# The second tile's rows, softmax and convolution moved earlier in the head of a fused convolution and two feed-forward layers

## The chip, the cores and the metric

The kernel runs on one core of a Trainium2 chip. The metric is the device time of one execution in microseconds, the median of some runs without a profile. The profile comes from one further execution.

## The reference

`x` is (2, 4096, 192), `weight_gen` is (2, 4096, 8, 7). Each token gets eight heads of seven weights, which a softmax normalises; the output of the first stage is a causal convolution over seven tokens with these weights. Two feed-forward layers follow, all in float32:

```
w = exp(weight_gen - max); w = w / (sum(w) + 1e-9)              # over the 7 taps
out[b,s,h,:] = sum_k w[b,s,h,k] * x_pad[b,s+k,h,:]              # 8 heads of 24 columns
h = max(out @ w_in, 0);  x1 = (h*h) @ w_out                     # 192 -> 2048 -> 192
h = x1 @ w_in2;          y  = (h*cos(h)) @ w_out2               # 192 -> 2048 -> 192
```

## The kernel before

The 8192 tokens are cut into 16 tiles of 512 (`TILES`, `TOK`). A tile is convolved and transposed, so that the 192 columns lie on partitions, and goes through the first layer in 16 chunks of 128 hidden columns (`SLOTS`); the second layer's chunks of the same tile run 19 slots behind (`LAG`). A slot `n` holds the up-projection of chunk `n` of layer 1, a down-projection of an earlier chunk of layer 1 and, from slot 19 on, the same for layer 2. To get float32 accuracy each operand is split into a high and a low half (`_hi`, `_lo`), and three products of halves are summed. TensorE does most matmuls on half of its rows, 64 each (`half`, L608).

Each engine has its own queue, in an order written out by hand in the loops over slots; semaphores tie them. In the first 19 slots (the head) there is no second layer, and the other engines have one-off work between the slots:

- **VectorE** starts with the softmax of `weight_gen` parts 0 and 1 (tiles 0 and 1), convolves tile 0 (`convolve_first`, L1426 and L1433), subtracts the first weight pieces' low halves (L1545, L1549) and makes the two low halves of x1 of tile 0 (L1553). Then per slot: the square of the relu (L1458, except for `ACT_SQUARES`, which ScalarE squares) and the low half of the chunk (`low`, L1507), and behind each slot what `CONV_AFTER` lists (the convolution of tile 1, `convolve_second`: products at L1401, sums at L1410, the running sum being in the PSUM tensor y1) and what `SOFTMAX_AFTER` lists (`softmax(part, op)`: op 0 the maximum, 1 the subtraction, 2 the sum, 3 add 1e-9 and take the reciprocal, 4 the scaling, L1387).
- **ScalarE** makes the relu, the high halves and the exponentials, and rounds the weight pieces (`piece_his`, L1126).
- **GpSimd** makes the low halves of the weight pieces (`piece_lo`: L562, L564, L566, L568 for each of 16 pieces), subtracts maxima (`shift`) and convolves the tiles from 2 on.
- **SP** issues most DMAs in one order: gen part group 0, rows of x of tile 0, weight pieces 0 to 3, gen group 1, the rows of tile 1 (`load_rows(1)`), pieces 4 and 5, gen group 2, further pieces. `load_rows(1)` waits until all seven products of `convolve_first` have read the same buffer `xc`, `load_rows(2)` for tile 1's last sum (`x1_ready`). `load_piece(pc)` waits until GpSimd is done with piece `pc - 4`.
- **TensorE** runs three chunks alone (`up_alone`: slots 0 to 2), then `head_slot`, which waits at its start for low n-3 of the chunk whose down-projection it holds (`downs_of_slot`: `g1_ready`). At the end of slot `turn_at(0)` it transposes tile 1 (`turn_x1`, L725, 16 instructions), for which it waits for `x1_ready`. `split_at(0)`, slot 13, is where ScalarE and VectorE split the transposed tile.

The first chunk uses x1's halves as they come (L635 to L652). Its waits on `x1_split` are for the two subtractions of VectorE at L1553; the matmul shown is L644:

```
pe.wait_ge(x1_hi_ready, 1)
...
pe.wait_ge(x1_split, 1)
pe.matmul(o, wa_hi[l][:, f_cols], xa_lo[l][:, par, :], start=False, stop=False)
...
pe.wait_ge(x1_split, 2)
```

Of the kernel before, what the change touches and what calls it, by code (L numbers as in the profile page):

```python
# [7 lines left out]
def conv_ffn_ffn_kernel(nc, x_d, gen_d, w_in1_d, w_out1_d, w_in2_d, w_out2_d, out_dram):  # L8
# [18 lines left out]
    SLOTS = FF // P  # L27
# [13 lines left out]
    TURN = 3  # L41
# [20 lines left out]
    PEEL = 2  # L62
# [20 lines left out]

    def turn_at(t):

        return (SLOTS - 3, SLOTS - 9)[t] if t < PEEL else TURN

    def split_at(t):

# [22 lines left out]
    with ctx:  # L112
# [137 lines left out]
        LATE = 4  # L250

        ACT_SQUARES = (2, 3, 4, 5, 6, 7, 8)
        CONV_SLOTS = (1, 1, 2, 2, 3, 4, 5, 6, 7, 8, 9, 10, 11)

# [7 lines left out]
        for k in range(TAPS):  # L264
            for op in range(2 if k else 1):
                CONV_AFTER.setdefault(CONV_SLOTS[2 * k - 1 + op if k else 0], []).append((k, op))

# [1 line left out]

        PARTS = [0] + [JJ * t for t in range(1, TILES + 1) if t == 1 or t % 2 == 0]  # L270
        LOADS = [0, 2, 5, len(PARTS) - 1]
        SOFTMAX_AFTER = {0: [(1, 2), (1, 3), (1, 4)]}
        SOFTMAX_AFTER.update({n: [(n - 1, 0)] for n in range(3, 10)})
        SOFTMAX_AFTER.update({12: [(2, 2)], 13: [(2, 3)]})
        SOFTMAX_IN = {29: [(3, 2)], 30: [(3, 3)]}
        SOFTMAX_IN.update({2 * SLOTS + (6, 7, 9, 10, 11, 12, 13, 14, 15, SLOTS + 6)[k]: [(4 + k // 2, 2 + k % 2)]
# [51 lines left out]
        def stat_view(part):  # L328
            a, b = gen_range(part)
            return stat[:, a * HEADS:b * HEADS]  # L330
# [44 lines left out]
        def load_first_own(eng, quarters):  # L375

            for q in quarters:
                eng.dma_start(xc[q * BLOCK:(q + 1) * BLOCK, HALO * DM:],  # L378
                              x_v[:, q * JJ * DM:(q + 1) * JJ * DM]).then_inc(x_own, 16)
# [31 lines left out]
        def store_a(eng, t, r, blocks):  # L411
            eng.wait_ge(out_a_ready, t + 1)
            tokens = slice(t * QUARTERS * JJ, (t + 1) * QUARTERS * JJ)
            for d in blocks:
                cols = slice(d * BLOCK, (d + 1) * BLOCK)
                eng.dma_start(out_v[:, tokens, cols],
                              out_a[r][cols, :].rearrange("n (j c) -> n j c", c=BLOCK)).then_inc(stored[r], 16)

        def store_d(eng, t, r, blocks):
            eng.wait_ge(out_d_ready, t + 1)  # L420
            half = QUARTERS * JJ // 2
            for k in blocks:
                j0 = t * QUARTERS * JJ + k * BLOCK // DD * half
                col = DA + k * BLOCK % DD
                eng.dma_start(out_v[:, j0:j0 + half, col:col + BLOCK],
                              out_d[r][k * BLOCK:(k + 1) * BLOCK, :].rearrange("n (j c) -> n j c", c=BLOCK)
                              ).then_inc(stored[r], 16)

        def load_gen(eng, r, quarters=range(QUARTERS)):
            part_a, part_b = LOADS[r], LOADS[r + 1]  # L430
            t0, t1 = PARTS[part_a] // JJ, PARTS[part_b] // JJ
            for q in quarters:
                eng.dma_start(gen[q * BLOCK:(q + 1) * BLOCK, PARTS[part_a] * GEN:PARTS[part_b] * GEN].rearrange(  # L433
                                  "p (t k) -> p t k", t=t1 - t0),
                              gen_v[:, t0:t1, q, :]).then_inc(gen_loaded[r], 16)

        @block.sync
        def _(sp):
            def load_piece(pc):
                l, q = divmod(pc, PL)  # L440
                r = pc % RING
                if pc >= RING:
                    sp.wait_ge(piece_ready[pc - RING], 3)
                cols = slice(q * PIECE, (q + 1) * PIECE)
                sp.dma_start(stage_a[:, r, :], w_in_d[l][0:DA, cols]).then_inc(piece_loaded[r], 16)
                sp.dma_start(stage_d[l * DD:(l + 1) * DD, r, :], w_in_d[l][DA:DM, cols]).then_inc(piece_loaded[r], 16)
                sp.dma_start(stage_o[:, r, :, :],
                             w_out_v[l][:, q * PF:(q + 1) * PF, :]).then_inc(piece_loaded[r], 16)

            def load_rows(c):  # L450
                if c == 1:
                    sp.wait_ge(first_product, TAPS)
                else:
                    sp.wait_ge(x1_ready, c - 1)
                sp.wait_ge(x_loaded, FIRST_X + NEXT_X * (c - 1))
                for q in range(QUARTERS):
                    at = ((c * QUARTERS + q) * JJ - HALO) * DM
                    sp.dma_start(xc[q * BLOCK:(q + 1) * BLOCK, :], x_v[:, at:at + ROWS * DM]).then_inc(x_loaded, 16)

            def move_blocks(t):  # L460

                sp.wait_ge(blocks_ready, t - 1)
                blocks = x_blocks[:, :].rearrange("p (j d n) -> p j d n", j=JJ, n=BLOCK)
                for d in range(DM // BLOCK):
                    for q in range(QUARTERS):
                        cols = slice(q * P, (q + 1) * P)
                        to = xt_a[d * BLOCK:(d + 1) * BLOCK, cols] if d < DA // BLOCK else \
                            xt_d[d * BLOCK - DA:(d + 1) * BLOCK - DA, cols]
                        sp.dma_start(to.rearrange("p (j n) -> p j n", j=JJ),
                                     blocks[q * BLOCK:(q + 1) * BLOCK, :, d, :]).then_inc(blocks_moved, 16)  # L470

            load_gen(sp, 0, (0, 1))
            load_first_own(sp, (0, 1))
            load_first_halo(sp, ((1, B), (0, 0), (0, 1), (1, 0), (1, 1)))
            for pc in range(RING):
                load_piece(pc)
            load_gen(sp, 1)
            load_rows(1)
            for pc in range(RING, RING + 2):
                load_piece(pc)  # L480
            load_gen(sp, 2)
            for pc in range(RING + 2, PL + 4):
                load_piece(pc)
            load_rows(2)
            for pc in range(PL + 4, PIECES):
                load_piece(pc)
            load_rows(3)
            move_blocks(2)
            for t in range(2, TILES + 2):
                if t + 2 < TILES:  # L490
                    load_rows(t + 2)
                if t + 1 < TILES:
                    move_blocks(t + 1)

                blocks = range(4 if t <= TILES else 2)
                store_a(sp, t - 2, t % 2, blocks)
                store_d(sp, t - 2, t % 2, blocks)
            for r in range(2):
                sp.wait_ge(stored[r], STORE * (TILES // 2))
# [802 lines left out]
        def _(dve):  # L1302
            def softmax(part, op):

                if op == 0:
                    dve.wait_ge(gen_loaded[sum(part >= a for a in LOADS[1:])], 16 * QUARTERS)
                    dve.tensor_reduce(stat_view(part), gen_view(part), axis=AX.X,
                                      op=ALU.max).then_inc(gen_max[part], 1)
                elif op == 1:
                    dve.wait_ge(gen_max[part], 1)  # L1310
                    dve.tensor_tensor(gen_view(part), gen_view(part), spread(part),
                                      ALU.subtract).then_inc(gen_shifted, 1)
                elif op == 2:
                    dve.wait_ge(gen_exp, part + 1)
                    dve.tensor_reduce(stat_view(part), gen_view(part), axis=AX.X,
                                      op=ALU.add).then_inc(gen_sum[part], 1)
                elif op == 4:
                    scale(part)
                else:
                    dve.wait_ge(gen_sum[part], 1)  # L1320
                    dve.tensor_scalar(stat_view(part), stat_view(part), 1e-9, None,
                                      ALU.add).then_inc(gen_sum[part], 1)
                    dve.wait_ge(gen_sum[part], 2)
                    dve.reciprocal(stat_view(part), stat_view(part)).then_inc(inv_ready, 1)
# [214 lines left out]
            for op in range(2, 4):  # L1539
# [8 lines left out]
            dve.wait_ge(piece_ready[0], 1)  # L1548
            dve.tensor_tensor(wd_lo[0:DD, 0:PIECE], stage_d[0:DD, 0, :], wd_hi[0:DD, 0:PIECE],  # L1549
                              ALU.subtract).then_inc(piece_ready[0], 1)  # L1550
            for part in range(2):
                dve.wait_ge(x1_hi_ready, part + 1)
                dve.tensor_tensor(by_half(x1_low(0, part)), x1_source(0, part), by_half(x1_high(0, part)),  # L1553
                                  ALU.subtract).then_inc(x1_split, 1)
            for n in range(TAIL):
# [4 lines left out]
                for k, op in CONV_AFTER.get(n, ()):  # L1560
                    convolve_second(k, op)
                for part, op in SOFTMAX_AFTER.get(n, ()):
                    softmax(part, op)
# [31 lines left out]
```

## Time and profile before

| | us |
|---|---|
| median of 3 runs | 1176.63 (1176.55 to 1176.8) |
| the profiled execution's own time | 1176.54 |
| its span, first to last instruction | 1174.7 |
| TensorE busy | 1167.3 (99%) |
| VectorE busy | 961.2 (82%) |
| ScalarE busy | 805.9 (69%) |
| GpSimd busy | 367.1 (31%) |

A span is the time from the first to the last instruction of the core; the execution's own time also has what lies around it. Shares are of the span. Engines overlap, so their busy times do not add up; the end of a matmul is modelled. The granted TensorE clock is 0.999 of full speed over the span.

### The profile page before, as it was taken

What the parts mean: (1) busy time and instruction counts of PE and PEld (TensorE: products, weight loads), DVE (VectorE), ACT (ScalarE), POOL (GpSimd) and SP (SyncE); (2) the same over time, 40 slices, a digit from 0 to 9 for tenths busy, and PEclk for the clock granted to TensorE, in tenths of its full rate; (3) what the DMA queues carried; (4) which work ended last, traced back from release to release, by engine and by line L of the source; (5) the groups of instructions that cost most, each with busy time, mean ns of one, the idle gap of its engine ahead of it and who ended that gap; (6) DMA issues with size and microseconds to landing.
All of it is one profiled execution on the core that took longest, in us unless ns stands there. A gap on an engine that the chain in (4) does not pass through costs nothing.

```text
span 1174.7 us, 25693 instructions
## 1 busy us (share of the span) xinstructions
PE 1167.3 (99%) x9906; PEld 1129.7 (96%) x9906; DVE 961.2 (82%) x1505; ACT 805.9 (69%) x1467; POOL 367.1 (31%) x265
## 2 busy tenths in 40 slices
PE   9999999999999999999999999999999999999998
PEld 7989999999999999999999999999999999999987
DVE  7968898878778787887878878787787878878787
ACT  5977766666666676666766666676666766666676
POOL 4994634070420606025070430705215070000000
PEclk9999999999999999999999999999999999999999
DMA  8511111110111101111011111101111000100001
GB/s 212 138 48 31 37 27 35 25 35 10 23 35 29 35 11 18 35 28 35 15 24 29 25 35 28 35 9 21 35 29 35 13 17 3 26 2 15 1 1 28
DMA packets 113173, 37.32 MB, mean 32 GB/s; under 512 B 101662, under 2 KB 110878, under 8 KB 113052
## 3 DMA queue, kind: packets, MB, share of 16 engines
q1 hardware_dynamic: 111100, 34.87, 14.3%
q8 instruction: 79, 1.29, 0.5%
q10 hardware_dynamic: 1952, 0.80, 0.3%
q14 instruction: 42, 0.34, 0.1%
HBM read 23.84 MB, written 6.29 MB: 26 GB/s over the span
## 4 chain that ended last, share of the span: by engine, by line
PE 99%; DVE 0%; ACT 0%; ACTq 0%; issue 0%
PE y L608 51%; PE h L608 46%; PE y L713 1%; PE h L637 0%; ACT L1131 0%; PE h L630 0%; PE y L674 0%; DVE tap L1426 0%; PE h L644 0%; PE h L640 0%; ACTq L378 0%; ACTq L389 0%; ACTq L433 0%; PE y L676 0%; PE y L675 0%
## 5 line engine op out<-in xcount | busy, mean ns | idle before, releaser
L608 PE MATMUL y<-g_hi,wo 64*128 64x512 f32 x3048 | 695.1, 393 | 0.2
L608 PE MATMUL y<-g_lo,wo 64*128 64x512 f32 x2032 | 515.9, 391 | 0.0
L608 PEld LDWEIGHTS y<-g_hi,wo 64*128 64x128 f32 x3048 | 414.3, 184 | 14.1 <-PE y L608 1.1
L529 POOL TENSOR_TENSOR tap<-xc,gen 128x768 f32<-128x768 f32 x98 | 151.3, 1550 | 575.4 <-DVE xd_lo L1513 555.3
L608 PEld LDWEIGHTS y<-g_lo,wo 64*128 64x128 f32 x2032 | 298.6, 184 | 1.7
L1167 ACT ACTIVATE turns<-turns 128x512 f32<-128x512 f32 x238 | 150.2, 631 | 182.6 <-DVE turns L1464 182.6
L608 PE MATMUL h<-xa_hi,wa_hi 64*128 64x512 f32 x1018 | 267.6, 397 | 0.1
L608 PE MATMUL h<-xa_hi,wa_lo 64*128 64x512 f32 x1018 | 262.7, 391 | 0.0
L608 PE MATMUL h<-xa_lo,wa_hi 64*128 64x512 f32 x1018 | 262.3, 391 | 0.0
L1484 DVE TENSOR_TENSOR h<-h,turns 128x512 f32<-128x512 f32 x238 | 165.6, 696 | 114.7 <-ACT turns L1167 114.2
L1458 DVE SCALAR_TENSOR_TENSOR h<-h,relu 128x512 f32<-128x512 f32 x249 | 173.4, 696 | 56.5 <-ACT relu L1142 54.3
L1180 ACT ACTIVATE g_hi<-h 128x512 fp32r<-128x512 f32 x238 | 142.6, 599 | 87.7 <-DVE h L1484 87.7
L1142 ACT ACTIVATE relu<-h 128x512 f32<-128x512 f32 x256 | 152.5, 596 | 62.8 <-PE h L608 62.2
L1494 DVE SCALAR_TENSOR_TENSOR g_lo<-h,g_hi 128x512 fp32r<-128x512 f32 x238 | 164.6, 692 | 18.8 <-ACT g_hi L1180 0.9
L1507 DVE TENSOR_TENSOR g_lo<-h,g_hi 128x512 fp32r<-128x512 f32 x256 | 174.3, 681 | 2.2 <-ACT g_hi L1192 1.2
L1464 DVE SCALAR_TENSOR_TENSOR turns<-h,turns 128x512 f32<-128x512 f32 x238 | 162.3, 682 | 1.4 <-ACT turns L1152 1.0
L1192 ACT ACTIVATE g_hi<-relu 128x512 fp32r<-128x512 f32 x256 | 158.0, 617 | 0.4
L608 PEld LDWEIGHTS h<-xa_lo,wa_hi 64*128 64x128 f32 x1018 | 149.1, 184 | 0.5
L608 PEld LDWEIGHTS h<-xa_hi,wa_lo 64*128 64x128 f32 x1018 | 149.2, 184 | 0.4
L1152 ACT ACTIVATE turns<-h 128x512 int32<-128x512 f32 x238 | 141.9, 596 | 1.2 <-PE h L608 1.2
L608 PEld LDWEIGHTS h<-xa_hi,wa_hi 64*128 64x128 f32 x1018 | 129.1, 184 | 12.3 <-issue 2.1
L608 PE MATMUL h<-xd_hi,wd_hi 64*128 64x512 f32 x513 | 133.3, 392 | 0.0
(124 smaller groups left out, 1076.0 us busy)
## 6 DMA issues: line engine op xcount, KB each, us to landing
xc<-in_x_dram SPq DMA_DIRECT2D x60, 240.0 KB
out_dram<-arena SPq DMA_DIRECT2D x62, 64.0 KB, 1.9
xt_a<-x_blocks SPq DMA_DIRECT2D x224, 16.0 KB, 1.8
arena<-in_moe_w_out_dram SPq DMA_DIRECT2D x16, 192.0 KB, 3.3
arena<-in_moe_w_in_dram SPq DMA_DIRECT2D x16, 128.0 KB, 2.6
out_dram<-arena SPq DMA_DIRECT2D x62, 32.0 KB, 1.7
xt_d<-x_blocks SPq DMA_DIRECT2D x112, 16.0 KB, 1.8
arena<-in_moe_w_in_dram SPq DMA_DIRECT2D x16, 64.0 KB, 2.9
```

What stands on the lines that cost most here:

```text
L529: pool.tensor_tensor(tap[:, k % 2, :].rearrange("p (r g) -> p r g", g=GROUP), rows[k], wk, ALU.mult).then_inc(pool_step, 1)
L608: return pe.matmul(o, w[rows, :], x[rows, :], start=start, stop=stop)
L1142: act.activation(relu[:, b, :], h1_bank(n), ACT.Relu).then_inc(relu_done, 1)
L1152: act.activation(turns[:, c, :], h2[c], ACT.Copy, bias=0.25).then_inc(turns_ready, 1)
L1167: act.activation(wave[:, c, :], wave[:, c, :], ACT.Sin, scale=2.0 * math.pi).then_inc(cos_ready, 1)
L1180: act.activation(g2_hi[:, c, :], h2[c], ACT.Copy, scale=2.0 * math.pi).then_inc(g2_hi_ready, 1)
L1192: act.activation(g1_buffers(n)[0], relu[:, n % 2, :], ACT.Square).then_inc(g1_hi_ready, 1)
L1458: dve.scalar_tensor_tensor(h1_bank(n), h1_bank(n), 0.0, relu[:, b, :], ALU.max, ALU.mult).then_inc(square_ready, 1)
L1464: dve.scalar_tensor_tensor(wave[:, c, :], h2[c], 0.25, turns[:, c, :], ALU.add, ALU.subtract).then_inc(fraction_ready, 1)
L1484: dve.tensor_tensor(h2[c], h2[c], wave[:, c, :], ALU.mult).then_inc(g2_made, 1)
L1494: dve.scalar_tensor_tensor(g2_lo[:, c, :], h2[c], 2.0 * math.pi, g2_hi[:, c, :], ALU.mult, ALU.subtract).then_inc(g2_ready, 1)
L1507: dve.tensor_tensor(lo, h1_bank(n), hi, ALU.subtract).then_inc(g1_ready, 1)
```

## The change

SP issues the rows of tile 1 ahead of gen group 1. VectorE does the last three softmax operations of part 1 (four instructions) before the low halves of tile 0's x1 instead of behind slot 0. The convolution of tile 1 begins behind slot 0 with three operations, has two behind slot 1 and one behind each of slots 2 to 9 (before: two behind slot 1, two behind slot 2, one behind each of slots 3 to 11). TensorE's transposes of tile 1 come behind slot 12 instead of 13.

```diff
     def turn_at(t):
 
-        return (SLOTS - 3, SLOTS - 9)[t] if t < PEEL else TURN
+        return (SLOTS - 4, SLOTS - 9)[t] if t < PEEL else TURN
...
-        CONV_SLOTS = (1, 1, 2, 2, 3, 4, 5, 6, 7, 8, 9, 10, 11)
+        CONV_SLOTS = (0, 0, 0, 1, 1, 2, 3, 4, 5, 6, 7, 8, 9)
...
-        SOFTMAX_AFTER = {0: [(1, 2), (1, 3), (1, 4)]}
-        SOFTMAX_AFTER.update({n: [(n - 1, 0)] for n in range(3, 10)})
+        SOFTMAX_AFTER = {n: [(n - 1, 0)] for n in range(3, 10)}
...
             for pc in range(RING):
                 load_piece(pc)
+            load_rows(1)
             load_gen(sp, 1)
-            load_rows(1)
...
             dve.tensor_tensor(wd_lo[0:DD, 0:PIECE], stage_d[0:DD, 0, :], wd_hi[0:DD, 0:PIECE],
                               ALU.subtract).then_inc(piece_ready[0], 1)
+            for op in range(2, 5):
+                softmax(1, op)
             for part in range(2):
                 dve.wait_ge(x1_hi_ready, part + 1)
```

## Rows read from the trace of the kernel before

**Rows 1.** The page, busy us, share of the span, instructions
```profile
PE 1167.3 (99%) x9906; PEld 1129.7 (96%) x9906; DVE 961.2 (82%) x1505; ACT 805.9 (69%) x1467; POOL 367.1 (31%) x265
```

**Rows 2.** Busy time by stretch: us from:to, length, busy of each engine, clock
```profile
22.00:62.00 40.00, 40.00 (x304) 36.02 (x304) 36.71 (x52) 35.88 (x74) 37.28 (x47) 1.00 0.66 158
62.00:75.00 13.00, 12.65 (x80) 9.04 (x79) 8.33 (x12) 10.22 (x18) 12.53 (x8) 1.00 0.10 28
75.00:1110.00 1035.00, 1035.00 (x8865) 1015.91 (x8867) 848.56 (x1326) 705.49 (x1276) 310.39 (x197) 1.00 0.12 24
```

**Rows 3.** Timeline of VectorE, 13 to 24 us: start, duration, line, operands, idle before
```profile
13.55 0.95 DVE L1426 TENSOR_TENSOR tap<-xc,gen 128x768 f32<-128x768 f32 x1
...
16.00 0.42 DVE L1549 TENSOR_TENSOR wd_lo<-arena,wd_hi 64x256 fp32r<-64x256 f32 x1
17.13 0.69 DVE L1553 TENSOR_TENSOR xa_lo<-y,xa_hi 128x512 fp32r<-128x512 f32 x1 [0.71 <-ACT xa_hi L1273]
...
20.71 0.69 DVE L1507 TENSOR_TENSOR g_lo<-h,g_hi 128x512 fp32r<-128x512 f32 x1
21.32 0.38 DVE L1315 TENSOR_REDUCE stat<-gen 128x32 f32<-128x224 f32 x1
...
22.38 0.39 DVE L1387 TENSOR_TENSOR gen<-gen,stat 128x224 f32<-128x224 f32 x1
22.69 0.69 DVE L1458 SCALAR_TENSOR_TENSOR h<-h,relu 128x512 f32<-128x512 f32 x1
23.42 0.69 DVE L1507 TENSOR_TENSOR g_lo<-h,g_hi 128x512 fp32r<-128x512 f32 x1
```

**Rows 4.** Line L1321 over the whole span: duration in ns, least, median, most
```profile
L1321 DVE TENSOR_SCALAR stat<-stat x9: 181/223/1573, 5.7 to 226.6; 128x64 f32<-128x64 f32 x7, 128x32 f32<-128x32 f32 x2
```

**Rows 5.** Timeline of TensorE: the first chunk's matmul of xa_lo
```profile
18.02 0.40 PE L644 MATMUL h<-xa_lo,wa_hi 128*128 128x512 f32 x1
```

**Rows 6.** Timeline of GpSimd, 16 to 26 us
```profile
16.50 0.72 POOL L562 TENSOR_TENSOR wa_lo<-arena,wa_hi 128x256 fp32r<-128x256 f32 x1 [13.93 <-DVE wd_lo L1549]
17.37 0.74 POOL L564 TENSOR_TENSOR wd_lo<-arena,wd_hi 64x256 fp32r<-64x256 f32 x1
18.08 0.45 POOL L566 TENSOR_TENSOR wo<-arena,wo 128x128 fp32r<-128x128 f32 x1
18.49 0.74 POOL L568 TENSOR_TENSOR wo<-arena,wo 128x256 fp32r<-128x256 f32 x1
...
22.06 0.46 POOL L566 TENSOR_TENSOR wo<-arena,wo 128x128 fp32r<-128x128 f32 x1
...
24.22 1.35 POOL L564 TENSOR_TENSOR wd_lo<-arena,wd_hi 64x256 fp32r<-64x256 f32 x1
```

**Rows 7.** Timeline of VectorE, 24 to 31 us
```profile
24.89 1.50 DVE L1401 TENSOR_TENSOR tap<-xc,gen 128x768 f32<-128x768 f32 x1
...
29.56 0.68 DVE L1507 TENSOR_TENSOR g_lo<-h,g_hi 128x512 fp32r<-128x512 f32 x1
30.16 0.95 DVE L1410 TENSOR_TENSOR y<-y,tap 128x768 f32<-128x768 f32 x1
```

**Rows 8.** Timeline of TensorE: first up-projection matmul of slots 4, 5 and 6
```profile
25.28 0.39 PE L608 MATMUL h<-xa_hi,wa_hi 64*128 64x512 f32 x1
...
27.85 0.39 PE L608 MATMUL h<-xa_hi,wa_hi 64*128 64x512 f32 x1
...
30.49 0.47 PE L608 MATMUL h<-xa_hi,wa_hi 64*128 64x512 f32 x1
```

**Rows 9.** Timeline of SP's queue: the gen loads and the rows of tile 1
```profile
12.25 3.23 SPq L433 DMA_DIRECT2D gen<-in_weight_gen_dram  x4
15.60 1.76 SPq L458 DMA_DIRECT2D xc<-in_x_dram  x4
```

**Rows 10.** Timeline: VectorE's last sum of tile 1, TensorE's transposes
```profile
49.74 0.95 DVE L1410 TENSOR_TENSOR x<-y,tap 128x768 f32<-128x768 f32 x1
...
50.96 0.67 PE L725 MATMUL y<-ident,x 64*128 64x64 f32 x14
```

## The prediction

> **What bounds the kernel now.** I read the page's busy shares first: TensorE is busy 1167.3 of 1174.7 us [rows 1]. Busy time by stretch comes next: from 22 to 62 us and from 75 to 1110 us it has no gap, 40.00 of 40.00 and 1035.00 of 1035.00 us [rows 2]. The order written out by hand is the same from 75 us on, so the change can act only on the head. There TensorE is a fixed chain of matmuls, and whatever delays one of them for lack of input stays in the end time: behind 22 us there is nothing idle to absorb it but 0.35 us between 62 and 75 us [rows 2], which is the second layer's starting chain. So the question is whether VectorE, which gives TensorE the low halves, is later or earlier than before for chunks 0 to 3. Times here are of the profiled execution: 1176.54 us, span 1174.7; the median of the plain runs is 1176.63, 0.09 more.
>
> I call "low n" the subtraction at L1507 that ends chunk n's low half. TensorE's slot n+3 needs low n.
>
> **How VectorE and GpSimd meet.** A product of 128x768 takes 0.95 us while GpSimd is idle (13.55 [rows 3]); the second product of tile 1 took 1.50 us, 24.89 to 26.39 [rows 7]. GpSimd's L564 takes 0.74 us alone and took 1.35, 24.22 to 25.57 [rows 6]. These fit one reading: only one of them runs at a time. L564 started while the first product ran and waited for it; the second product then waited for L564 until 25.44, which is 0.13 before L564's reported end, and ran its 0.95 to 26.39. Subtractions and additions with an operand in PSUM do not wait (low 3 at 29.56, 0.68; the addition at 30.16, 0.95, GpSimd being busy beside both [rows 7]). The small TENSOR_SCALAR at L1321 took 181 ns at best and 1573 at worst [rows 4], so it waits too, with one operand only.
>
> The Trainium skill, "SBUF — State Buffer", section "SBUF: two separate sides", calls the port pair that VectorE and GpSimd share "an exclusive lock, not a bandwidth split", taken by a VectorE operation with two SBUF inputs or in a two-port mode. The rows above agree. Without such a lock the sum below would be 0.9 us; with it, it is 2.9. That the lock speaks against this change is my main reason.
>
> **Softmax ahead of the low halves of x1 (adds four operations, takes them from slot 0).** VectorE sits between wd_lo (16.00) and xa_lo (17.13) with 0.71 us idle [rows 3], waiting for ScalarE. The four operations took, start to start, 21.32 to 22.69 = 1.37 us (the last, 22.38, overlaps the next by 0.08) [rows 3]. Without GpSimd: they start at 16.34 (wd_lo's 0.42 less 0.08 overlap), so xa_lo starts at 17.71, 0.58 late. With the lock: GpSimd's L562 runs 16.50 to 17.22 and L564 17.37 to 18.11 [rows 6]. The TENSOR_SCALAR, due at 16.76, waits until 17.09 and ends at 17.27; the reciprocal runs 17.31 to 17.66; the scaling multiply, due at 17.70, waits for L564 until 17.98 and ends at 18.37. xa_lo then starts at 18.29, 1.16 late. TensorE's L644 started at 18.02, 0.20 behind xa_lo's end at 17.82 [rows 3, 5], and all that follows is in its queue. **Term 1: +1.16 us (bounds 0.58 and 1.16).** What the cover was worth: 0.71 of the softmax is hidden, the rest is paid by the first chunk. Chunk 1 gains from it, since the softmax stood between its low 0 and low 1, but nothing waited there.
>
> **Three convolution operations in slot 0, two in slot 1.** Before, low 0 (20.71) was followed by the softmax, square 1 and low 1 (23.42 to 24.11) [rows 3]; slot 4 began at 25.28 [rows 8]. From low 3 (ends 30.24) to the matmul at 30.49 [rows 7, 8] the handover takes 0.25 us; slots are 2.57 apart when nothing waits (25.28 to 27.85) and slot 6 was 2.64 behind slot 5 [rows 8], followed by a restart that costs 0.08 more. So slot 4 had 25.28 - 24.36 = 0.92 in hand.
> Now walk it, GpSimd's list shifted by 0.14 (the scaling multiply holds L566 back from 18.08 to 18.22 [rows 6]):
> - Low 0 starts at 20.71 + 1.16 = 21.87, the first product is due 0.61 later, 22.48. L566 (22.06 + 0.14 = 22.20) holds the port until 22.53. Product 22.53 to 23.48.
> - GpSimd's L568, 0.74 us, came at 22.61 and waited to 23.33; it lets go at 23.94. Second product to 24.89.
> - The addition of two SBUF buffers needs both (24.93); L562 has gone ahead at 24.74 until 25.34. Addition to 26.29.
> - Square 1 from 26.21, low 1 0.73 later, 26.94 to 27.63. Slot 4 can begin at 27.88; without the wait it would at 25.28 + 1.16 = 26.44. **Term 2: +1.44, and 0.08 for the restart.** Lower bound, three operations unstretched (0.86, 0.99, 0.86 start to start): with term 1 at 0.58, low 1 ends at 26.03, slot 4 waits 0.42 + 0.08.
> - Slot 1: the product is due at 27.55, waits for L566 and L568 (27.43) until 28.04, ends 28.99; the addition into PSUM 29.03 to 29.98; low 2 29.89 to 30.58. Slot 5 at 30.83 against 27.88 + 0.08 + 2.57 = 30.53. **Term 3: +0.30 and 0.08** (bounds: nothing, 0.4).
> - Slot 2 has one operation where it had two: low 3 starts at 31.36, ends 32.05; slot 6 is due at 30.83 + 2.65 = 33.48, so it does not wait. **Term 4: -0.16**, the stall and restart of slot 6 before.
> From slot 3 the operations are one per slot as before, two slots ahead, and low 4 has over a microsecond in hand.
> Sum: 1.16 + 1.52 + 0.38 - 0.16 = **+2.9 us**.
>
> **Rows of x ahead of weight_gen.** SP issued the four gen loads in 12.25 to 15.48 and the rows in 15.60 to 17.36 [rows 9]. Now SP stands at the wait for the seventh product, which ends at 13.55 + 0.95 = 14.50 [rows 3]: 2.25 us in which nothing is issued, behind it the gen loads, piece 4 and all later pieces. Rows go out at 14.6 to 16.4, gen to 19.6, piece 4 from 19.7. The landing of rows has no row of its own. Before, the first product (right behind low 1's 0.61 us, so 24.03) found them landed, at most 6.7 us behind the last issue at 17.36; now that bound gives 23.0 against the need at 22.48: cost 0 to 0.5, and I take 0, since the queue ahead is shorter. gen is first read behind slot 3, about 32 us: nothing. Piece 4 comes a few tenths later; ScalarE, which converts it, is not what low 3 waits for now. Cost 0, at most 0.3.
>
> **Transposes behind slot 12 instead of 13.** Tile 1's last sum ended at 49.74 + 0.95 = 50.69, and the 16 transposes began at 50.96 [rows 10], where TensorE had just run out of the slot's matmuls: 0.02 of handover room, no stall. The same 16 instructions are paid one slot earlier. The sum now ends two slots earlier, some 47 us, ahead of their place at about 51. 0 us (bounds -0.3, +0.1). Chunk 13's result comes half a microsecond later to ScalarE, which runs behind there anyway. The second tile's rows (load_rows(2), behind this sum) go out earlier, which nothing waited for.
>
> **Rivals.**
> 1. *The first product gets the port first.* If term 1 is 0.65 (the scaling multiply slips in ahead of L564), the product is due at 21.97, before L566. The same walk gives product to 22.92, second to 24.05, addition to 25.46, low 1 to 26.80, slot 4 at 27.05 against 25.93: 1.12 + 0.08; slot 5 is not late. 0.65 + 1.20 - 0.16 = +1.7: 1178.3 us. For it: two instructions 0.3 us apart decide. Against it: L564 had a start 0.33 ahead.
> 2. *No stretching at all*: 0.58 + 0.50 - 0.16 = +0.9: 1177.5. Against it the 1.50 and 1.35 us rows.
> 3. *Larger*: the rows are late by 0.5, or one more operation is held by GpSimd (0.5): +3.4: 1180.0.
> 4. *Other side*: the extra 0.5 us around the transposes was partly a wait for the sum. Slots 13 and 14 would have to give back more than the head costs; the price is at most 0.3 there and 0.16 at slot 6, and it decides only if the head costs less than 0.46, that is if the softmax hides wholly in the 0.71 idle: 1176.2. Against it 1.37 > 0.71.
>
> **Numbers.** Forecast 1176.6 + 2.9 = 1179.5 us, chance 0.52; rival 1 0.24, rival 2 0.12, rival 3 0.09, rival 4 0.03. What a measurement here can tell from no change is about 0.2%, 2.35 us. The forecast's own range, 1179.1 to 1180.0, lies above 1178.98 nearly whole; slower by over that 0.58, within it 0.41, faster 0.01. Range 1177.6 to 1180.2.
>
> **What would show it.** xa_lo at 18.3 instead of 17.13, L644 at 19.2; L1321 and L1387 longer than 0.2 and 0.39. The first product at 22.5, low 1 ending near 27.6, TensorE waiting 1.4 us before slot 4 for L1507. Slot 6 some 3.0 later than 30.49, and the same shift at the end. Wrong if the products beside GpSimd keep 0.95, if slot 4 does not wait, or if the shift at slot 6 is given back later.

## The result: slower by 8 us, by an operation that took nine times its length, and by the clock

| | median us | runs, us |
|---|---|---|
| before | 1176.62 | 1176.37 to 1177.24 (6) |
| changed | 1184.58 | 1181.36 to 1186.49 (6) |
| ratio | 1.0064 | 95% interval 1.0053 to 1.0075 |

The forecast was 1179.5 (range 1177.6 to 1180.2). The sign came out as forecast, the size did not, and the runs now spread over 5 us where they had spread over 1. Line numbers after 272 are one lower in the changed kernel (L1386 is L1387 before).

The page's busy shares look like those of [rows 1]:

```profile
PE 1170.9 (99%) x9906; PEld 1130.2 (96%) x9906; DVE 963.6 (82%) x1505; ACT 806.2 (68%) x1467; POOL 366.6 (31%) x265
```

TensorE is busy 3.6 us more with the same matmuls, the first hint. VectorE ahead of the first chunk, in the changed kernel's timeline (start, duration, line, operands, idle before):

```profile
16.17 0.42 DVE L1548 TENSOR_TENSOR wd_lo<-arena,wd_hi 64x256 fp32r<-64x256 f32 x1
16.51 0.37 DVE L1314 TENSOR_REDUCE stat<-gen 128x32 f32<-128x224 f32 x1
16.92 0.51 DVE L1320 TENSOR_SCALAR stat<-stat 128x32 f32<-128x32 f32 x1
17.47 0.35 DVE L1323 RECIPROCAL stat<-stat 128x32 f32<-128x32 f32 x1
17.86 1.17 DVE L1386 TENSOR_TENSOR gen<-gen,stat 128x224 f32<-128x224 f32 x1
19.06 0.69 DVE L1554 TENSOR_TENSOR xa_lo<-y,xa_hi 128x512 fp32r<-128x512 f32 x1
```

GpSimd at the same time:

```profile
17.54 0.73 POOL L563 TENSOR_TENSOR wd_lo<-arena,wd_hi 64x256 fp32r<-64x256 f32 x1
18.24 0.45 POOL L565 TENSOR_TENSOR wo<-arena,wo 128x128 fp32r<-128x128 f32 x1
18.65 0.96 POOL L567 TENSOR_TENSOR wo<-arena,wo 128x256 fp32r<-128x256 f32 x1
```

The scaling multiply, 0.39 us long in [rows 3], took 1.17: it stood from 17.86 until 18.64 (19.03 less 0.39) and was passed by L565. So xa_lo began at 19.06, against 17.13 [rows 3]. TensorE:

```profile
19.80 0.50 PE L643 MATMUL h<-xa_lo,wa_hi 128*128 128x512 f32 x1 [1.39 <-DVE xa_lo L1554]
...
21.13 0.79 PE L636 MATMUL h<-xa_hi,wa_hi 128*128 128x512 f32 x1
...
24.28 0.79 PE L636 MATMUL h<-xa_hi,wa_hi 128*128 128x512 f32 x1
...
30.14 0.39 PE L607 MATMUL h<-xa_hi,wa_hi 64*128 64x512 f32 x1
...
35.27 0.39 PE L607 MATMUL h<-xa_hi,wa_hi 64*128 64x512 f32 x1
```

The first row answers to [rows 5]: 19.80 against 18.02, 1.78 late, behind a gap of 1.39 us. The last two answer to [rows 8]: slot 4 is 4.86 late, slot 6 4.78, and the span is 4.7 longer (1179.4 against 1174.7). Between the first chunk and slot 4 another 3.08 us went, but not by waiting: the matmuls grew to 0.79 us. Busy time and granted clock by stretch (from:to, length, busy of PE, PEld, DVE, ACT, POOL, then the clock) show why:

```profile
19.00:20.00 1.00, 0.20 (x1) 0.19 (x1) 0.97 (x3) 0.37 (x1) 1.00 (x3) 1.00 0.85 169
20.00:21.00 1.00, 1.00 (x4) 0.48 (x3) 0.34 (x1) 0.00 (x0) 1.00 (x3) 1.00 1.06 217
21.00:22.00 1.00, 1.00 (x3) 0.78 (x3) 0.14 (x1) 0.73 (x2) 0.86 (x2) 0.54 1.14 223
...
27.00:28.00 1.00, 1.00 (x8) 0.80 (x6) 0.96 (x3) 0.46 (x1) 1.00 (x2) 0.55 1.13 215
28.00:29.00 1.00, 1.00 (x8) 0.77 (x6) 1.00 (x2) 0.97 (x3) 0.20 (x1) 1.00 1.12 237
```

From 21.1 to 27.9 us (0.54 and 0.55 being mixtures) the granted clock is 0.50, that is 1.2 GHz instead of 2.4. TensorE counts as wholly busy there; only the clock column gives it away. A share of busy time would have hidden it.

This profile is of the fastest of the six executions. What the others lost is the first question to the experiments.

### The profile page after: what moved, and what is told of

It is laid out like the page before. It is cut to its first block, busy times and chain, and to the rows that moved or that the text cites. A ratio compares the mean times of both kernels' runs of the same rounds, so it can differ in the third digit from the quotient of the medians.

```text
span 1179.4 us, 25693 instructions
## 1 busy us (share of the span) xinstructions
PE 1170.9 (99%) x9906; PEld 1130.2 (96%) x9906; DVE 963.6 (82%) x1505; ACT 806.2 (68%) x1467; POOL 366.6 (31%) x265
## 4 chain that ended last, share of the span: by engine, by line
PE 98%; DVE 1%; DMA 0%; SPq 0%; issue 0%; ACT 0%; DVEq 0%
PE y L607 51%; PE h L607 46%; DMA xc<-in_x_dram 0%; DVE tap L1425 0%; PE h L636 0%; PE h L643 0%; SPq L391 0%; DVE gen L1386 0%; PE h L639 0%; DVE tap L1432 0%; PE y L673 0%; DVE turns L1432 0%; DVE relu L1425 0%; DVE turns L1425 0%; SPq L377 0%
```

## The experiments

Theory A: the softmax ahead of xa_lo makes TensorE wait, and the gap lets the clock fall. Theory B: the early convolution makes the loss. After the first four runs theory A got a third part, called C: VectorE gets the shared port only in a pause of GpSimd's work. A filler is a matmul whose result nobody reads (L629, `keep_busy`).

| kernel | median us (range, runs) | ratio to before, 95% |
|---|---|---|
| softmax ahead, nothing else changed | 1185.62 (1184.38 to 1187.35, 4) | 1.0075 (1.006 to 1.009) |
| changed, softmax behind the low halves | 1181.40 (1181.25 to 1182.71, 5) | 1.0038 (1.0023 to 1.0052) |
| changed, 6 fillers | 1184.70 (1183.32 to 1186.26, 4) | 1.0066 (1.0051 to 1.0081) |
| changed, GpSimd starts behind the multiply | 1178.39 (1178.24 to 1179.06, 10) | 1.0013 (1.0004 to 1.0023) |
| changed, a gap in GpSimd's work | 1179.39 (1179.08 to 1182.32, 7) | 1.0027 (1.0015 to 1.0038) |
| softmax ahead, GpSimd starts behind the multiply | 1178.01 (1177.59 to 1178.32, 10) | 1.0008 (0.9998 to 1.0017) |
| changed, 17 fillers | 1181.37 (1181.32 to 1181.64, 5) | 1.0036 (1.0023 to 1.0049) |
| rows of x first, nothing else | 1176.71 (1176.40 to 1177.54, 10) | 1.0000 (0.999 to 1.0009) |
| changed, twice more | 1184.57, 1187.24 | |
| early convolution without the softmax's move | 1182.15 (1181.42 to 1183.12, 4) | 1.0044 (1.0029 to 1.0059) |
| transposes earlier, nothing else | 1178.18 (1177.79 to 1181.32, 10) | 1.0015 (1.0005 to 1.0024) |

The kernel before ran beside them at 1176.85, 1176.87 and 1176.98 us.

**1. Only the softmax moved.**

```diff
-        SOFTMAX_AFTER = {0: [(1, 2), (1, 3), (1, 4)]}
...
+            for op in range(2, 5):
+                softmax(1, op)
             for part in range(2):
                 dve.wait_ge(x1_hi_ready, part + 1)
```

> The kernel before with one part of the change: the three softmax operations of part 1 stand ahead of the low halves of x1; rows, convolution and transposes are where they were. Theory A (the head's wait and the clock): TensorE waits for xa_lo 1.3 to 1.8 us longer than before, and the granted clock then falls to half for about 6 us, which costs another 3 us or more: 1181 to 1185 us, all or nearly all of the change's loss. Theory B (the early convolution and its wait ahead of slot 4 make the loss, and the clock fell because of the sum of waits): here at most the wait for xa_lo, +1.8 us, 1178.4 us, clock 0.999.

1185.62 us: theory A (0.6 us above its range). The move of four small operations alone loses as much as the whole change. Its timeline has the multiply and what TensorE then waited, and the stretch from 23 to 36 us the clock, 0.50 throughout:

```profile
17.61 3.54 DVE L1386 TENSOR_TENSOR gen<-gen,stat 128x224 f32<-128x224 f32 x1
...
21.93 0.51 PE L643 MATMUL h<-xa_lo,wa_hi 128*128 128x512 f32 x1 [3.77 <-DVE xa_lo L1554]
```

```profile
23.00:36.00 13.00, 13.00 (x42) 8.64 (x42) 7.71 (x9) 6.34 (x12) 6.03 (x9) 0.50 0.77 173
```

I had expected at most 1.8 us of waiting here; it was 3.8. The multiply can wait much longer than in the first profile.

**2. The changed kernel twice more.** No edit.

> The changed kernel, unaltered, for one more profile. Theory C says that its first profile (1181.4 us, the multiply at L1386 taking 1.17 us) was one of the short waits and that most executions have the long one: near 1184.5 us, the multiply 3.5 us, TensorE's gap near 3.7 us, the granted clock at half for over 10 us. If the other executions lost their time elsewhere, the multiply is again near 1.2 us and the gap near 1.4.

> The same once more, with the same expectations: the multiply near 3.5 us and 1184.5 us in most executions, near 1.2 us and 1181.4 us in a few.

Both had the long wait. From the first of them, VectorE's multiply, GpSimd beside it, and TensorE:

```profile
17.81 3.53 DVE L1386 TENSOR_TENSOR gen<-gen,stat 128x224 f32<-128x224 f32 x1
18.20 0.44 POOL L565 TENSOR_TENSOR wo<-arena,wo 128x128 fp32r<-128x128 f32 x1
18.61 0.71 POOL L567 TENSOR_TENSOR wo<-arena,wo 128x256 fp32r<-128x256 f32 x1
19.29 0.45 POOL L565 TENSOR_TENSOR wo<-arena,wo 128x128 fp32r<-128x128 f32 x1
19.70 0.71 POOL L567 TENSOR_TENSOR wo<-arena,wo 128x256 fp32r<-128x256 f32 x1
20.38 0.71 POOL L561 TENSOR_TENSOR wa_lo<-arena,wa_hi 128x256 fp32r<-128x256 f32 x1
21.24 0.72 POOL L563 TENSOR_TENSOR wd_lo<-arena,wd_hi 64x256 fp32r<-64x256 f32 x1
22.12 0.80 PE L643 MATMUL h<-xa_lo,wa_hi 128*128 128x512 f32 x1 [3.81 <-DVE xa_lo L1554]
```

The multiply ended at 21.34, so it was let in at 20.95: just when L561 (20.38 to 21.09) was done. Behind L561 there is a pause of 0.15 us, since L563 waits for L561's own semaphore. The five instructions from 18.20 to 20.38 follow each other without any, and all of them passed the waiting multiply. The two executions differ in the clock: half from 20.6 to 30.8 us in the first (1184.57), from 20.0 to 37.1 in the second (1187.24), worked out from the shares of single microseconds. The first stands at the median of the six runs, 1184.58, so of the typical loss 4.1 us is waiting (22.12 against 18.02), and the other 3.9 us arises behind it, where the clock is at half.

**3. A gap in GpSimd's work.** The same instructions in the same order; GpSimd only waits for its own L563 before L565.

```diff
                 piece_lo(1, op)
+            pool.wait_ge(piece_ready[1], 2)
             piece_lo(0, 2)
```

> The changed kernel with one more wait on GpSimd: behind L563 of piece 1 it waits for that instruction's own semaphore before L565 of piece 0, which leaves the sequence of instructions as it is but opens a gap of some 0.15 us between the two. Theory C (VectorE gets the shared port only in a gap between GpSimd's instructions, and GpSimd's back-to-back instructions keep it): the multiply at L1386 is let in at that gap, takes 0.4 to 0.8 us instead of 1.2 to 3.6, xa_lo starts near 18.3, TensorE's gap is about 0.7 us, and the time is 1178.0 to 1180.0 us. If arbitration is by chance or by order of arrival, the multiply varies as before and the median stays at 1182 to 1186 us.

```profile
17.29 0.74 POOL L563 TENSOR_TENSOR wd_lo<-arena,wd_hi 64x256 fp32r<-64x256 f32 x1
18.10 0.49 POOL L565 TENSOR_TENSOR wo<-arena,wo 128x128 fp32r<-128x128 f32 x1
...
17.60 0.67 DVE L1387 TENSOR_TENSOR gen<-gen,stat 128x224 f32<-128x224 f32 x1
...
19.05 0.50 PE L644 MATMUL h<-xa_lo,wa_hi 128*128 128x512 f32 x1 [0.85 <-DVE xa_lo L1555]
27.82 0.47 PE L608 MATMUL h<-xa_hi,wa_hi 64*128 64x512 f32 x1 [1.24 <-DVE g_lo L1507]
33.25 0.39 PE L608 MATMUL h<-xa_hi,wa_hi 64*128 64x512 f32 x1
```

As theory C said: the multiply takes 0.67, and 5.2 us of the median are back (1184.58 to 1179.39), by one semaphore wait that adds no work. The multiply and L565 both wait for L563 here, and the multiply goes first. In this profile L644 is 1.03 late, slot 4 2.54, slot 6 2.76. Three of the seven runs had a mean clock of 0.995 to 0.997 and took 1180.5 to 1182.3: the clock still fell now and then.

So a pause is enough at this place. As a rule theory C does not hold: elsewhere a waiting VectorE operation was let in where GpSimd makes no pause. In the kernel before:

```profile
26.67 0.73 POOL L568 TENSOR_TENSOR wo<-arena,wo 128x256 fp32r<-128x256 f32 x1
26.91 1.32 DVE L1410 TENSOR_TENSOR y<-tap 128x768 f32<-128x768 f32 x1
27.37 1.45 POOL L562 TENSOR_TENSOR wa_lo<-arena,wa_hi 128x256 fp32r<-128x256 f32 x1
```

In the kernel with only the rows of x first (experiment 7), where it is the same multiply behind slot 0:

```profile
22.50 0.74 POOL L568 TENSOR_TENSOR wo<-arena,wo 128x256 fp32r<-128x256 f32 x1
22.59 0.90 DVE L1387 TENSOR_TENSOR gen<-gen,stat 128x224 f32<-128x224 f32 x1
23.19 0.89 POOL L562 TENSOR_TENSOR wa_lo<-arena,wa_hi 128x256 fp32r<-128x256 f32 x1
```

In both, GpSimd's next instruction was issued without a pause and was the one held (1.45 and 0.89 us instead of 0.73). Of some hundred such waits of VectorE between 14 and 80 us in the fourteen profiles, all but seven ended at GpSimd's first change of instruction, a third of them without a pause. The seven are the softmax operations beside GpSimd's first row of instructions, from 17.6 to 21.2 us. What sets that row apart was not tested.

**4. GpSimd starts behind the multiply**, in the changed kernel and in experiment 1's.

```diff
             pool.wait_ge(piece_ready[0], 2)
+            pool.wait_ge(gen_scaled, 2)
```

> The changed kernel with GpSimd's first piece work waiting until the softmax's scaling multiply has ended. Theory A, with the shared port as the cause of the long softmax: the multiply at L1386 takes 0.39 us instead of 1.17 and the TENSOR_SCALAR at L1320 0.18 instead of 0.51; xa_lo starts near 17.9 instead of 19.06, TensorE's gap is 0.4 to 0.6 us instead of 1.39. If so short a gap leaves the clock alone, 1177.5 to 1179 us; if it falls all the same, 1180 to 1184 us. If GpSimd is not the cause, the multiply still takes over 1 us.

> The kernel before with the softmax operations ahead of the low halves of x1 and GpSimd's first piece work waiting for the scaling multiply; rows, convolution and transposes as before. Theory C with the early convolution as a second, separate cost: L644 starts 0.4 us later than before and slot 4 does not wait, 1176.9 to 1177.4 us; the difference to the changed kernel with the same wait on GpSimd (1178.4) is the price of the early convolution, 1.0 to 1.5 us. If the convolution's place costs nothing, it is 1178.4 here too.

In the changed kernel:

```profile
16.62 0.18 DVE L1321 TENSOR_SCALAR stat<-stat 128x32 f32<-128x32 f32 x1
...
17.23 0.39 DVE L1387 TENSOR_TENSOR gen<-gen,stat 128x224 f32<-128x224 f32 x1
...
18.39 0.49 PE L644 MATMUL h<-xa_lo,wa_hi 128*128 128x512 f32 x1 [0.21 <-DVE xa_lo L1555]
27.24 0.47 PE L608 MATMUL h<-xa_hi,wa_hi 64*128 64x512 f32 x1 [1.31 <-DVE g_lo L1507]
```

With GpSimd idle both operations have their short durations, L644 is 0.37 late, and all ten runs keep the clock (0.999 or 1.0). What is left of the loss, 1.6 us, arises at slot 4: 27.24 is 1.96 late.

The second kernel was to give the early convolution's price by difference. It does not: at 1178.01 it is only 0.4 us better, and above what I expected. L644 was 0.58 late in its profile. Slot 6 was 0.63 late there, so slot 4 did not wait, as expected; but the second layer's first chunk was 1.76 late (70.64 against 68.88), again behind a VectorE operation held by GpSimd, further on:

```profile
68.55 2.04 DVE L1531 TENSOR_TENSOR xd_lo<-y_part,xd_hi 64x512 fp32r<-64x512 f32 x1
...
70.64 0.50 PE L637 MATMUL h<-xa_hi,wa_hi 128*128 128x512 f32 x1 [0.68 <-DVE xd_lo L1531]
```

L1531 has two SBUF operands and took 2.04 us instead of 0.69, beside one 1.54 us instruction of GpSimd's convolution of tile 2, which had started 0.05 us earlier. The 1.6 us at slot 4 are read from the slot, not from the two medians.

**5. Fillers, to take away TensorE's gap but not its wait.**

```diff
                 if first:
-                    keep_busy(1)
+                    keep_busy(17)
                     pe.wait_ge(x1_split, 1)
```

> The changed kernel with six filler matmuls instead of one in front of the first chunk's wait for xa_lo (five more of 0.23 us, some 1.2 us, in what was a 1.4 us gap). Theory A, with the gap in TensorE's work as the cause of the clock's fall: the clock stays at 1.0 through 17 to 30 us though xa_lo comes as late; lost are 1.8 us of waiting and 0.3 to 1.4 us ahead of slot 4: 1178.7 to 1179.8 us. If the clock falls for another reason, it falls here too and the time is 1181 to 1185 us.

> The changed kernel with 17 filler matmuls instead of one ahead of the wait for xa_lo, 3.7 us more of them. Theory C: the multiply at L1386 takes as long as before (up to 3.6 us), so the first chunk is still some 3.8 us late, but TensorE has nearly no gap; if the gap is what lets the granted clock fall, it stays at 1.0 and the time is 1180.0 to 1181.8 us. If the clock falls all the same, 1184 to 1187 us.

With 6 (`keep_busy(6)` at the same place) the time was in the range expected if the clock falls for another reason, but the run cannot tell: the multiply took 3.55 us in its profile, a gap of 2.56 us was left, and the clock fell behind it. With 17:

```profile
17.59 3.61 DVE L1386 TENSOR_TENSOR gen<-gen,stat 128x224 f32<-128x224 f32 x1
...
21.97 0.50 PE L643 MATMUL h<-xa_lo,wa_hi 128*128 128x512 f32 x1 [0.18 <-DVE xa_lo L1554]
30.25 0.47 PE L607 MATMUL h<-xa_hi,wa_hi 64*128 64x512 f32 x1 [0.74 <-DVE g_lo L1506]
```

and the same stretch table for 17 to 30 us:

```profile
17.00:30.00 13.00, 12.14 (x56) 8.23 (x54) 11.27 (x13) 7.57 (x17) 8.99 (x15) 1.00 1.09 236
```

xa_lo is 3.95 late as in experiment 2, the clock is 1.00 all through, and all five runs lie within 0.4 us. 1184.58 to 1181.37: on balance the clock costs 3.2 us of the typical loss, and the scatter was its too. Slot 4 now waits 1.0 us more (30.25 - 25.28 - 3.95), which the slow clock had covered; in the main this is why 3.2 is less than the 3.9 of experiment 2.

**6. Softmax between the low halves and slot 0.** The changed kernel with the two lines below the loop instead of above it.

```diff
-            for op in range(2, 5):
-                softmax(1, op)
             for part in range(2):
...
+            for op in range(2, 5):
+                softmax(1, op)
```

> The changed kernel, but with the three softmax operations behind the low halves of x1 and ahead of slot 0. Theory A: TensorE's first chunk is as before (L644's matmul near 18.0 us), the clock stays at 1.0, and what is left is VectorE's first slots: 0 to 0.3 us from the softmax running into square 0, and 0.4 to 1.4 us in front of slot 4: 1176.9 to 1178.3 us. Theory B: no better than the changed kernel, 1181 to 1185 us.

The first chunk was as before, but the 1.5 us of idle VectorE did not hold the softmax: now the TENSOR_SCALAR stood behind four of GpSimd's instructions in a row, square 0 and low 0 came late, and slot 4 waited 2.48 us, in which the clock fell to 0.50:

```profile
18.81 2.33 DVE L1320 TENSOR_SCALAR stat<-stat 128x32 f32<-128x32 f32 x1
...
28.92 0.76 PE L607 MATMUL h<-xa_hi,wa_hi 64*128 64x512 f32 x1 [2.48 <-DVE g_lo L1506]
```

Theory A's range (to 1178.3) was missed by 3 us, by the same error as in experiment 1: I had the operation wait for one instruction at most.

**7. The other parts alone.**

```diff
+                if n == 0:
+                    for op in range(2, 5):
+                        softmax(1, op)
                 for k, op in CONV_AFTER.get(n, ()):
```

is the changed kernel with the softmax back behind slot 0;

```diff
+            load_rows(1)
             load_gen(sp, 1)
-            load_rows(1)
```

is the kernel before with the rows first, and the last one is the kernel before with `turn_at(0)` at slot 12.

> The changed kernel with the softmax operations back behind slot 0, ahead of the convolution's first three operations there: rows, convolution and transposes as changed, the first chunk as before. The head's wait is gone; low 1 is late by the softmax (1.4 us) and three operations (2.7 to 3.7 us), so TensorE waits 2.3 to 3.6 us in front of slot 4. If the clock stays: 1178.8 to 1180.4 us; if a gap this long lets it fall, as the gap ahead of the first chunk did, 1182 to 1184 us. If the early convolution costs nothing: 1176.9 us.

> The kernel before with only the DMA order changed: rows of tile 1 ahead of gen group 1. All theories: nothing waits for either, 1176.4 to 1177.2 us, no difference that can be told. If the rows' place mattered (a later piece 4 holding up ScalarE and slot 6), 1177.5 us or more.

> The kernel before with the transposes of tile 1 behind slot 12 instead of 13, all else as it was. The convolution still ends two operations later than slot 9, behind slot 11, at about 50.7 us, which is 2.3 us after slot 12's place at 48.4: TensorE waits for it, 1178.6 to 1179.2 us. This tells that the transposes could not have been moved without the convolution. If TensorE does not wait, 1176.9 us.

The first matmul of slot 4 in the first, and of the transposes in the last:

```profile
28.74 0.47 PE L607 MATMUL h<-xa_hi,wa_hi 64*128 64x512 f32 x1 [3.16 <-DVE g_lo L1506]
```

```profile
50.94 0.37 PE L725 MATMUL y<-ident,x 64*128 64x64 f32 x2 [2.29 <-issue]
```

The early convolution costs by itself when the softmax stands behind slot 0: slot 4 waits 3.16 us and the clock falls (0.50 at 30 to 31 us), 1182.15 us. The rows' order costs nothing. The transposes could only move because the convolution had; alone they wait 2.29 us, and in some of the ten runs the clock falls behind that too (1177.8 with it at 1.0, up to 1181.3 at 0.998). The median, 1178.18, is below the expected 1178.6 to 1179.2: in the runs at full clock less than half of the 2.29 us shows in the time, and where the rest is regained stays open.

## Why the prediction was wrong

- **What bounds the kernel** was right: all of the loss arises ahead of 38 us, and slot 6's shift (4.78 in the profile) is the end's (4.7). Nothing was given back.
- **The shared port** was read rightly as exclusive, and as holding the one-operand TENSOR_SCALAR (0.51 forecast 0.51: due at 16.92, let in when L561 ended).
- **Term 1 is the step that failed**: "the scaling multiply, due at 17.70, waits for L564 until 17.98". It took for granted that the waiting operation is next when the running instruction ends. Instead GpSimd's L565, L567, L565, L567 and L561 followed without a pause and went first: 3.5 us in five of six profiles with the multiply ahead of xa_lo and GpSimd's sequence untouched, 1.17 in the other. Term 1 measured 1.8 to 4.3 us for 1.16. With a pause of 0.15 us at that place (experiment 3) the multiply took 0.67 and L644 was 1.03 late, and the rest of the sum followed: slot 4 2.54 late (2.60 plus 0.08 forecast), the end 2.6 (2.9), 1179.4 us (1179.5). In the kernel before, each wait of this kind ended at GpSimd's first change of instruction, without a pause too (26.91 above), so the rule was taken from true cases; none of them stood beside GpSimd's first row of instructions. Why the rule fails there stays open.
- **The clock has no term in the prediction**, which is its second error, 3.2 us at the median. I priced a gap as its own length. The kernel before has no gap of over 0.4 us between 17 us and its last matmul, so no row there showed what one does. Experiment 5 shows it: the same wait for xa_lo with the gap filled keeps the clock.
- **Terms 2 and 3**, the wait ahead of slot 4 (1.44 and 0.08) and 5: in the changed kernel's own profile slot 4 does not wait (4.86 of its 4.86 us are older), because TensorE at half speed no longer outruns VectorE. Where the clock stayed, the wait was there: 1.5 us in experiment 3, 1.6 in 4, 1.0 in 5. Slot 5's 0.38 was 0.2 in experiment 3. So term 2 was right, term 3 somewhat high, and both were hidden by a larger one.
- **Term 4, the rows, the transposes** came out as forecast: slot 6 lost no time (2.56 behind slot 5 in the changed kernel), the rows alone have a ratio of 1.0000, and the transposes did not wait in the changed kernel.
- **The range** took its upper end from one more held operation, 0.5 us. The longest row at hand was larger: [rows 4] showed 1.57 us for an operation of 0.18 (there held by one GpSimd instruction of 1.86 us). Even that would have been less than the 3.1 us that the multiply waited.

## What to carry to other kernels

A VectorE operation with two SBUF operands (or a TENSOR_SCALAR in SBUF), placed beside a row of GpSimd instructions without waits between them, can be passed by several of them: allow for the length of that row, keep the operation off the path, start GpSimd's work behind it, or open a gap for it by letting GpSimd wait on itself. Price a stall of TensorE with the clock behind it; look at the granted clock by microsecond, since busy shares hide it. Filler matmuls buy the clock back if they leave nearly no gap (17 did, 6 did not). In the head of a kernel an idle slot on one engine is not free room if its neighbour owns the port.

## What the runs showed of the hardware

- VectorE's TENSOR_TENSOR of 128x224, 0.39 us alone, took up to 3.61 us beside GpSimd, and the TENSOR_SCALAR of 128x32, 0.18 us alone, up to 2.33. In these cases they were let in at GpSimd's pause of about 0.15 us, after five and three of its instructions had passed. In the changed kernel's first profile the multiply got in between L565 and L567, and in the other places (experiment 3) at the first change of instruction, where there was often no pause. What decides was not settled. The Trainium skill, "SBUF — State Buffer", section "Who interferes with whom", says that whoever issues first has the pair for the whole instruction and the other fully blocks; the rows agree, and show besides that the blocked one is not always the next in turn.
- The granted clock fell to 0.50 at gaps of TensorE of 1.39 us (the changed kernel's first profile), 2.29 us (transposes earlier, 0.50 from 51 to 54 us) and 3.81 us (experiment 2), and stayed at half for about 3 to 17 us, through which TensorE was mostly busy. Behind a gap of 1.31 us it stayed at 1.00 (experiment 4), and runs of one kernel can do either (experiment 3). The fall comes within the gap (20.6 us in experiment 2, ahead of 22.12) or behind it (21.1 us in the changed kernel's first profile, the gap ending at 19.80).
- With the clock's fall the head's stall turned a spread of 1 us between executions into one of 5 to 6.
